# Attention's kv products in two blocks, its loads on one queue, the expert choice per batch, and token numbers from two engines

## The chip, the cores and the metric

The kernel runs on one core of a Trainium2 chip. The metric is the device time of one execution in microseconds (us); of several runs the median counts. Each compute engine (PE is TensorE, DVE is VectorE, ACT is ScalarE, POOL is GpSimd) and SP (SyncE) runs its own instruction stream in order; streams meet at semaphores. SP, ACT and POOL each have a DMA queue.

## The reference

The work has three parts: linear attention with a norm over each head, a mixture of experts in which every token takes its best expert, and a second one in which experts have a capacity and tokens are assigned by descending logit.

```python
# q, k, v: (8 batches, 8 heads, 576 rows, 64), float32
kv = np.einsum('bhsd,bhse->bhde', k, v)
out = np.einsum('bhsd,bhde->bhse', q, kv)
rms = np.sqrt(np.mean(out * out, axis=-1, keepdims=True) + 1e-06)
x = out / rms * g_norm                       # then (4608 tokens, 512)

# first mixture, 8 experts, 512 -> 1024 -> 512
logits = x @ w_gate
e_idx = np.argmax(logits, axis=1)
gate_w = softmax(logits)[np.arange(N), e_idx]
eom = 1.0 / (1.0 + np.exp(-(x @ w_output_gate)))
out[mask] = gate_w * eom[e] * (np.maximum(x[mask] @ w1[e], 0) @ w2[e])
# second mixture: the same shapes, at most N // 8 tokens an expert,
# tokens assigned greedily over all (token, expert) logits in descending order
```

## The kernel before

**Attention.** The rows of a batch lie on 96 partitions, six rows each (`CT = 6`). PE walks `STEPS_A = 56` steps; with `B = 8` batches, batch b's work begins in step 6b. In a step (lines 658 to 714) PE does in this order: a group of eight products k by v, 1/6 of the batch's kv (L670, profile name kv_ps, 16 matmul records, as each float32 product is two); in one step of six the gates of kv (L682, kt_ps, waits for ACT's kvT); the turning of a row tile of q, 7 steps behind (L692, qt_ps); the product of q with kv, 8 steps behind (L704, o_ps); in one step of six the turning of kv (L713, kt_ps, waits for ACT's copies of kv, L1001). So kv of batch b is made in steps 6b to 6b+5, its turning comes in step 6b+6, and its products with q in steps 6b+8 to 6b+13. In the text below, "step c of a batch" counts its products with q.

ACT per step: the copy of the turned q (L1007), the regrouping of the next q (L1015, named q), and, behind DVE's scaling of the product (xrow, L1207), the squares (L1027) and the copy of the raw logits (L1031). DVE: the scaling, the sums of squares (L1186), and once a batch the inverse root (L1225 to 1229), the scaled logits (lraw, L1240) and their sum (lgs, L1244). POOL then scales xrow in two runs of three instructions (L586) and stores each half to x_rows (L592). DVE's L1207 waits in steps 0 and 3 of a batch until the store of the same half two batches before has landed (L1206).

**Loads.** k and v of a batch come in halves of four heads, 576 KB each, into two buffers each; q comes in halves into three. SP issues the k halves and one q half (lines 470 to 475), waiting for the kv products that free the buffer; ACT issues the v halves and the other q half (L972 to 990), the first seven before its other work and the rest inside its steps. All go through `load_heads` (L459). Behind the last of them SP issues the first expert's weights (L493). ACT splits these weights after attention (`first_high`, L965).

**Routing.** After the last batch DVE takes, over all 48 row tiles (`G1`) at once, the largest logit (L1251), the shifted logits for ACT's exponentials (L1253), the one-hot choice with ties to the lower expert (L1255 to 1259), a running count (L1262), the gate factor (L1269 to 1274), and each token's slot in a list sorted by expert (L1279 to 1292). Then, in three equal thirds of 16 row tiles, it makes a one-hot of the slot's tile (oha1, L1296), two products of it with the two digits of the token number (ra1, L1299; 64 times the one plus the other), and a one-hot of the place within the tile (ohb and ohx, L1305 to 1308). PE multiplies these (L727), and DVE joins the digits to the token numbers tok_i and the mask cap_v (L1322 to 1326) and releases `s_route`. On it wait POOL's gathers of x (L604), SP, and PE's first mixture. Both mixtures follow; the change leaves them alone.

## Time and profile before

| what | us |
|---|---|
| median of 3 runs | 1430.93 |
| the runs | 1423.6 to 1432.06 |
| the profiled execution | 1435.5 |
| its span | 1433.8 |
| PE busy in the span | 1264.1 (88%) |
| DVE busy | 975.6 (68%) |
| ACT busy | 443.4 (31%) |
| POOL busy | 384.1 (27%) |

The span runs from the first to the last instruction of the one profiled execution; 1.7 us of that execution lie around it. All rows below come from it, with times counted from the span's start. A share of busy time is an average over attention, routing and two mixtures, which have different limits, so the rows below are taken from the first 230 us, where the change is.

### The profile page before, as it was taken

How to read it: one execution, taken by the hardware profiler on the slowest of the kernel's cores; microseconds unless marked ns; L12 is line 12 of the kernel's file. 1: busy time of each engine (PE TensorE's matmuls, PEld its weight loads, DVE VectorE, ACT ScalarE, POOL GpSimd, SP SyncE). 2: the span in 40 equal slices, each digit the busy share in tenths (PEclk: the TensorE clock that was granted, in tenths of full speed). 3: DMA queues.
4: the chain of work that ended last, by engine and by line, in shares of the span. 5: the costliest groups of instructions: out<-in, count | busy, mean ns of one | idle time of the engine just before them, and what ended most of it. 6: DMA issues, size and time to landing. Idle time of an engine off the chain costs nothing.

```text
span 1433.8 us, 21814 instructions
## 1 busy us (share of the span) xinstructions
PE 1264.1 (88%) x7584; PEld 1013.6 (71%) x7584; DVE 975.6 (68%) x2318; ACT 443.4 (31%) x801; POOL 384.1 (27%) x323
## 2 busy tenths in 40 slices
PE   5987925999799999999999317999999999999996
PEld 4876814788688888888888215677777777777884
DVE  1464696476576777777668787788888788886621
ACT  1665641222222222222222021232333333233421
POOL 2233442955460725436000001020211111111110
PEclk7899866999999999999999657999999999999998
DMA  9999224698331432433110031313232332314100
GB/s 212 229 284 306 83 71 162 230 341 294 95 124 49 151 110 90 154 88 127 45 38 23 15 117 34 125 56 129 75 125 90 108 102 84 133 59 145 47 30 19
DMA packets 71014, 172.07 MB, mean 120 GB/s; under 512 B 11752, under 2 KB 30264, under 8 KB 70272
## 3 DMA queue, kind: packets, MB, share of 16 engines
q1 hardware_dynamic: 37104, 94.45, 20.6%
q10 hardware_dynamic: 21696, 36.35, 9.1%
q0 software_dynamic: 12112, 39.87, 8.7%
q8 instruction: 68, 1.11, 0.3%
q14 instruction: 34, 0.28, 0.1%
HBM read 129.42 MB, written 41.23 MB: 119 GB/s over the span
## 4 chain that ended last, share of the span: by engine, by line
PE 70%; DVE 8%; DMA 8%; POOL 7%; issue 5%; ACT 1%; SPq 0%; POOLq 0%; ACTq 0%; DVEq 0%
PE bank L742 52%; PE bank L814 4%; PE bank L760 4%; DMA v_sb<-in_v 3%; POOL w_lo L578 3%; PE bank L870 2%; POOL xrow L586 2%; DMA xst<-x_rows,tok_i 2%; PE bank L807 2%; PE o_ps L704 1%; POOL w_hi L576 1%; DMA w_sb<-in_moe_w 1%; DMA x_rows<-xrow 1%; POOL xst L604 1%; PE bank L797 1%
## 5 line engine op out<-in xcount | busy, mean ns | idle before, releaser
L1386 DVE SCALAR_TENSOR_TENSOR bank<-bank,factor,wg2b 128x512 f32<-128x512 f32 x336 | 254.6, 758 | 10.4
L1352 DVE TENSOR_TENSOR hT_lo<-bank,hT_hi 128x512 fp32r<-128x512 f32 x150 | 96.5, 684 | 169.9 <-ACT hT_hi L1092 154.5
L1049 ACT ACTIVATE h<-bank 128x512 f32<-128x512 f32 x166 | 99.1, 598 | 320.3 <-PE bank L742 305.5
L742 PE MATMUL bank<-w_hi,xT_hi 128*128 (+1 forms) x600 | 175.7, 415 | 10.2 <-POOL w_lo L578 7.3
L742 PE MATMUL bank<-w_lo,xT_hi 128*128 (+1 forms) x600 | 174.3, 406 | 0.0
L633 POOL DMA_INDIRECT xg<-y_rows,gat_i x40 | 39.5, 987 | 495.4 <-DVE sca_i L1509 382.2
L742 PE MATMUL bank<-w_hi,xT_lo 128*128 (+1 forms) x600 | 168.1, 401 | 0.0
L742 PE MATMUL bank<-w_hi,hT_hi 128*128 (+1 forms) x600 | 160.9, 409 | 5.2 <-DVE score L1389 3.3
L742 PE MATMUL bank<-w_lo,hT_hi 128*128 (+1 forms) x600 | 158.2, 400 | 0.0
L742 PE MATMUL bank<-w_hi,hT_lo 128*128 (+1 forms) x600 | 155.7, 398 | 0.0
L578 POOL TENSOR_TENSOR w_lo<-w_sb,w_hi 128x1024 fp32r<-128x1024 f32 x56 | 134.2, 2396 | 4.5
L742 PEld LDWEIGHTS bank<-w_hi,xT_lo 128*128 128x128 f32 x600 | 113.4, 191 | 27.0
L742 PEld LDWEIGHTS bank<-w_lo,xT_hi 128*128 128x128 f32 x600 | 112.5, 191 | 26.6
L742 PEld LDWEIGHTS bank<-w_hi,hT_lo 128*128 128x128 f32 x600 | 111.7, 188 | 26.7
L742 PEld LDWEIGHTS bank<-w_hi,xT_hi 128*128 128x128 f32 x600 | 107.6, 192 | 31.3 <-issue 11.4
L742 PEld LDWEIGHTS bank<-w_lo,hT_hi 128*128 128x128 f32 x600 | 111.1, 189 | 25.5
L742 PEld LDWEIGHTS bank<-w_hi,hT_hi 128*128 128x128 f32 x600 | 109.3, 192 | 27.4 <-issue 6.7
L576 POOL CAST w_hi<-w_sb 128x1024 fp32r<-128x1024 f32 x56 | 58.2, 1040 | 182.6 <-DMA w_sb<-in_moe_w 182.6
L1056 ACT ACTIVATE y<-bank,factor 128x512 f32<-128x512 f32 x43 | 29.6, 687 | 216.5 <-PE bank L742 191.7
L814 PEld LDWEIGHTS bank<-ident,h 128*128 128x128 f32 x664 | 86.4, 190 | 7.6 <-ACT h L1049 0.4
L1092 ACT ACTIVATE hT_hi<-bank 128x512 fp32r<-128x512 f32 x150 | 81.5, 597 | 25.5 <-PE bank L814 16.0
L640 POOL DMA_INDIRECT out<-y,sca_i x40 | 39.8, 995 | 180.8 <-ACT y L1080 118.9
(257 smaller groups left out, 1809.3 us busy)
## 6 DMA issues: line engine op xcount, KB each, us to landing
w_sb<-in_moe_w SPq DMA_DIRECT2D x112, 512.0 KB, 7.6
y_rows<-y ACTq DMA_DIRECT2D x43, 256.0 KB
x_sorted<-xst SPq DMA_DIRECT2D x41, 260.0 KB
xg<-x_sorted ACTq DMA_DIRECT2D x41, 260.0 KB
k_sb<-in_k SPq DMA_DIRECT2D x16, 576.0 KB, 12.6
v_sb<-in_v ACTq DMA_DIRECT2D x16, 576.0 KB, 14.1
x_rows<-xrow POOLq DMA_DIRECT2D x16, 576.0 KB, 5.4
w_sb<-in_moe_w SPq DMA_DIRECT2D x4, 2048.0 KB, 14.4
```

What stands on the lines that cost most here:

```text
L576: pool.tensor_copy(w_hi[:, 1 - e % 2, cols(i)], w_sb[:, e % 2, cols(i)]).then_inc(s_phi, 1)
L578: pool.tensor_tensor(w_lo[:, e % 2, cols(i)], w_sb[:, e % 2, cols(i)], w_hi[:, 1 - e % 2, cols(i)].bitcast(F32), ALU.subtract).then_inc(s_ ...
L633: pool.indirect_dma_start(out=xgs[w % 2][0:rows, 0:DM], out_offset=None, in_=y_rows[:, :], in_offset=bass.IndirectOffsetOnAxis(ap=gat_i[0: ...
L640: pool.indirect_dma_start(out=out[:, :], out_offset=bass.IndirectOffsetOnAxis(ap=sca_i[0:rows, w:w + 1], axis=0), in_=ys[w % 2][0:rows, :] ...
L742: mm = pe.matmul(ps, a[:, i % chunks, :], b[:, i % chunks, cols], start=(i == 0), stop=(i == 3 * chunks - 1))
L760: mm = pe.matmul(ps[0:rows, :], act[:, c, 0:rows], w[rows < P][:, c, cols], start=(i == 0), stop=(i == 2 * chunks - 1))
L814: mm = pe.transpose(th_ps[half][:, i * P:(i + 1) * P], h[:, half * 4 + i:F:FC], ident[:, :])
L1049: act.activation(h[:, half * HALF:(half + 1) * HALF], h_ps[half][:, :], ACT.Copy if short else ACT.Relu).then_inc(s_h, 1)
L1056: act.activation(ys[t % 2][:, :], y1_ps[t % 2][:, :], ACT.Copy, scale=factor[:, t:t + 1]).then_inc(s_y, 1)
L1092: act.activation(hT_hi[:, half * 4:(half + 1) * 4, :].rearrange("p a b -> p (a b)"), th_ps[half][:, :], ACT.Copy).then_inc(s_hT, 1)
L1352: dve.tensor_tensor(hT_lo[:, half * 4:(half + 1) * 4, :].rearrange("p a b -> p (a b)"), th_ps[half][:, :], hT_hi[:, half * 4:(half + 1) * ...
L1386: ch.link(dve.scalar_tensor_tensor(out=prod_ps[:, :], in0=y1_ps[t % 2][:, :], scalar=factor[:, t:t + 1], in1=wg2b[:, e, :], op0=ALU.mult, ...
```

## The change

Four things change. (1) SP issues all loads of q, k and v in the order k, v, k, v, q, with q of a batch in one transfer of 1152 KB; ACT issues none. (2) After batch 0, the kv of batch b is made in two blocks of three groups, in steps 1 and 3 of the products of batch b - 1. (3) The largest logit, the shifted logits and the one-hot choice are made per batch in DVE's steps 4 and 5 behind its logits, on 6 row tiles at a time; the exponentials still run once, after the last batch. (4) Token numbers are split as (row of the partition, middle of the batch and step): one factor is a number per partition (row1), so ACT makes its product with a scaled copy, and DVE makes the other; the parts have 20, 16 and 12 row tiles; `s_route` is released behind tok_i, ahead of the mask.

```diff
+        MIDDLE = S * B // 2 - PT * CT // 2
...
-        payload1 = sb("payload1", [PT, G1, 2], F16)
+        payload1 = sb("payload1", [PT, G1], F16)
+        row1 = sb("row1", [PT, 1])
...
+        ROUTED = [slice(0, 20), slice(20, 36), slice(36, G1)]
+        N_CONST = 10
...
+        KV_BESIDE = ((), (0, 1, 2), (), (3, 4, 5), (), ())
+
+        def kv_steps(s):
+
+            if s < LAG_T:
+                return [(0, s)]
+            e, c = at_step(s, LAG_O)
+            return [(e + 1, i) for i in KV_BESIDE[c]] if e is not None and e + 1 < B else []
...
                     wait_pos(sp, s_kv, (b - 2) * 2 + n + 1)
-                    load_heads(sp, k, k_sb[b % 2], b, n, s_kvl[b % 2][n])
+                    for src, dst in ((k, k_sb), (v, v_sb)):
+                        sp.dma_start(dst[b % 2][:, n * half:(n + 1) * half, :],
+                                     src[b, n * half:(n + 1) * half].rearrange("h (p c) d -> p h (c d)", c=CT)
+                                     ).then_inc(s_kvl[b % 2][n], 16)
                 wait_pos(sp, s_q2, (b - 2) * CT)
-                load_heads(sp, q, q_sb[b % 3], b, 0, s_ql[b % 3])
+                sp.dma_start(q_sb[b % 3][:, :, :], q[b].rearrange("h (p c) d -> p h (c d)", c=CT)).then_inc(s_ql[b % 3], 16)
...
-                if b < B:
+                for b, i in kv_steps(s):
                     if i % 3 == 0:
                         pe.wait_ge(s_kvl[b % 2][i // 3], (b // 2 + 1) * 32)
...
-            for b in range(2):
-                for n in range(2):
-                    load_v(b, n)
-                load_q(b)
-            load_q(2)
             for s in range(STEPS_A + 1):
-                b, i = divmod(s, CT)
-                if i % 3 == 0 and 0 <= b - (i == 0) < B - 2:
-                    load_v(b + 2 - (i == 0), 1 - i // 3)
-                if i == 0 and 3 <= b + 1 < B:
-                    load_q(b + 1)
...
+            for n, gs in enumerate(ROUTED):
+                act.wait_ge(s_oha, n + 1)
+                act.activation(ra1[:, gs, :, 1], oha1[:, gs, :], ACT.Copy, scale=row1[:, 0:1]).then_inc(s_rar, 1)
             act.wait_ge(s_wgt, 1)
...
-            for s in range(STEPS_A + 4):
+            for s in range(STEPS_A + 6):
...
+                if e is not None and c >= 4:
+                    of = slice(e * CT, (e + 1) * CT)
+                    lg, mxb, part = lgs[:, of, 0:E], mx[:, of].unsqueeze(2).to_broadcast([PT, CT, E]), oh[:, of, :]
+                    if c == 4:
+                        dve.wait_ge(s_lgs, e + 1)
+                        link(dve.tensor_reduce(mx[:, of], lg, AX, ALU.max))
+                        ch.inc(dve.tensor_tensor(part, lg, mxb, ALU.is_equal))
+                        dve.tensor_tensor(sh[:, of, :], lg, mxb, ALU.subtract).then_inc(s_sh, 1)
+                        ch.wait()
+                        link(dve.tensor_tensor(part, part, rank8[0:PT, :].unsqueeze(1).to_broadcast([PT, CT, E]), ALU.mult))
+                    if c == 5:
+                        dve.wait_ge(s_sh, e + 1)
+                        link(dve.tensor_reduce(mx[:, of], part, AX, ALU.max))
+                        ch.inc(dve.tensor_tensor(onehot[:, :, of].rearrange("p e g -> p g e"), part, mxb, ALU.is_equal))
+                        link(dve.tensor_tensor(part, part, mxb, ALU.is_equal))
...
+                dve.wait_ge(s_oha, ROUTED.index(gs) + 1)
                 ch.wait()
...
+                dve.tensor_tensor(ra1[:, gs, :, 0], oha1[:, gs, :],
+                                  payload1[:, gs].unsqueeze(2).to_broadcast([PT, n_all, T1]), ALU.mult).then_inc(s_ohb, 1)
```

On PE, at the start of attention, before (kv_ps is the kv products, qt_ps the turned q, o_ps the product of q with kv, kt_ps the turned kv and its gates):

```order
0 L656 UNCONDITIONAL_BRANCH
1 L670 MATMUL kv_ps<-v_sb,k_sb 64x64 x56
2 L713 MATMUL kt_ps<-ident,kvgb 128x128 x4
3 L670 MATMUL kv_ps<-v_sb,k_sb 64x64 x8
4 L682 MATMUL kt_ps<-gate_bd,kvT 128x32 x4
5 L692 MATMUL qt_ps<-ident,q 128x96 x4
6 L670 MATMUL kv_ps<-v_sb,k_sb 64x64 x8
7 L692 MATMUL qt_ps<-ident,q 128x96 x4
8 L704 MATMUL o_ps<-kvgb,qT 96x160 x4
9 L670 MATMUL kv_ps<-v_sb,k_sb 64x64 x8
10 L692 MATMUL qt_ps<-ident,q 128x96 x4
```

And the same place now:

```order
1 L682 MATMUL kv_ps<-v_sb,k_sb 64x64 x48
2 L725 MATMUL kt_ps<-ident,kvgb 128x128 x4
3 L694 MATMUL kt_ps<-gate_bd,kvT 128x32 x4
4 L704 MATMUL qt_ps<-ident,q 128x96 x8
5 L716 MATMUL o_ps<-kvgb,qT 96x160 x4
6 L682 MATMUL kv_ps<-v_sb,k_sb 64x64 x24
7 L704 MATMUL qt_ps<-ident,q 128x96 x4
8 L716 MATMUL o_ps<-kvgb,qT 96x160 x4
9 L704 MATMUL qt_ps<-ident,q 128x96 x4
10 L716 MATMUL o_ps<-kvgb,qT 96x160 x4
11 L682 MATMUL kv_ps<-v_sb,k_sb 64x64 x24
```

The first kv group of batch 1 stood ahead of the turning of batch 0's kv; now the first product with q comes ahead of any kv of batch 1, and its groups stand in blocks of 24 products.

On DVE, behind the last logits, before (mx is the largest logit, sh the shifted ones, oh the one-hot in the making):

```order
184 L1244 TENSOR_REDUCE lgs<-lraw 96x96
185 L1251 TENSOR_REDUCE mx<-lgs 96x48
186 L1253 TENSOR_TENSOR sh<-lgs,mx 96x384
187 L1255 TENSOR_TENSOR oh<-lgs,mx 96x384
188 L1256 TENSOR_TENSOR oh<-oh,rank 96x384
189 L1257 TENSOR_REDUCE mx<-oh 96x48
190 L1258 TENSOR_TENSOR oh<-oh,mx 96x384
191 L1259 COPY onehot<-oh 96x384
192 L1262 SCALAR_TENSOR_TENSOR inc<-segment,onehot 96x384
```

And now:

```order
231 L1239 TENSOR_REDUCE lgs<-lraw 96x96
232 L1247 TENSOR_REDUCE mx<-lgs 96x6
233 L1248 TENSOR_TENSOR oh<-lgs,mx 96x48
234 L1249 TENSOR_TENSOR sh<-lgs,mx 96x48
235 L1251 TENSOR_TENSOR oh<-oh,rank 96x48
236 L1254 TENSOR_REDUCE mx<-oh 96x6
237 L1255 TENSOR_TENSOR onehot<-oh,mx 96x6x8
238 L1256 TENSOR_TENSOR oh<-oh,mx 96x48
239 L1259 SCALAR_TENSOR_TENSOR inc<-segment,onehot 96x384
```

Seven operations remain between the last logits and the running count, each on an eighth of the elements; the other seven batches' share lies in the steps of attention.

## Rows read from the trace of the kernel before

**Rows 1.** Stretches: PE, PEld, DVE, ACT, POOL busy us, granted clock, DMA share, GB/s.

```profile
20.00:40.00 20.00, 14.18 (x121) 12.78 (x122) 1.83 (x4) 7.06 (x14) 0.00 (x0) 0.66 1.10 229
76.00:78.00 2.00, 2.00 (x23) 1.73 (x22) 0.00 (x0) 0.00 (x0) 0.00 (x0) 1.00 1.03 406
160.00:180.00 20.00, 16.89 (x145) 14.94 (x144) 14.32 (x26) 13.47 (x34) 8.23 (x8) 0.91 0.21 61
```

**Rows 2.** Waits of 0 to 240 us: total us, times, longest.

```profile
DVE xrow L1207 <- DMA x_rows<-xrow: 12.7, 2, 8.8
...
ACT L1001 <- issue: 20.9, 1, 20.9
PE kv_ps L670 <- DMA v_sb<-in_v: 20.5, 4, 8.7
```

**Rows 3.** PE in order of time: start, us, instructions, in brackets its wait.

```profile
15.26 3.94 PE L670 MATMUL kv_ps<-v_sb,k_sb 96*64 96x64 f32 x48 [2.56 <-DMA v_sb<-in_v]
25.82 1.57 PE L670 MATMUL kv_ps<-v_sb,k_sb 96*64 96x64 f32 x16 [6.62 <-DMA v_sb<-in_v]
27.32 1.12 PE L713 MATMUL kt_ps<-ident,kvgb 128*128 128x128 f32 x4
...
36.58 0.97 PE L670 MATMUL kv_ps<-v_sb,k_sb 96*64 96x64 f32 x16
...
93.89 0.93 PE L670 MATMUL kv_ps<-v_sb,k_sb 96*64 96x64 f32 x16
...
96.31 0.97 PE L670 MATMUL kv_ps<-v_sb,k_sb 96*64 96x64 f32 x16
...
106.84 0.66 PE L713 MATMUL kt_ps<-ident,kvgb 128*128 128x128 f32 x4 [0.64 <-ACT kvgb L1001]
...
108.35 1.08 PE L682 MATMUL kt_ps<-gate_bd,kvT 128*128 128x32 f32 x8
...
110.81 0.93 PE L670 MATMUL kv_ps<-v_sb,k_sb 96*64 96x64 f32 x16
```

**Rows 4.** Batch 7's steps, which have no kv beside them, in order of time.

```profile
175.37 1.63 PE L704 MATMUL o_ps<-kvgb,qT 128*96 128x160 f32 x8
...
179.08 0.69 DVE L1207 TENSOR_TENSOR xrow<-o_ps,g_sb 96x512 f32<-96x512 f32 x1 [0.55 <-PE o_ps L704]
...
181.51 0.55 PE L692 MATMUL qt_ps<-ident,q 96*128 96x96 f32 x4
...
186.43 1.33 PE L704 MATMUL o_ps<-kvgb,qT 128*96 128x160 f32 x8 [0.59 <-ACT qT L1007]
```

**Rows 5.** DMA: packets at 24 to 34 us; q1 (SP's) at 105 to 107; a store at 124.

```profile
DMA packets 1540, 2.30 MB, mean 230 GB/s; under 512 B 54, under 2 KB 1539, under 8 KB 1539
...
q1 hardware_dynamic: 321, 0.47, 101.9%
...
x_rows<-xrow POOLq DMA_DIRECT2D x1, 576.0 KB, 15.6
```

**Rows 6.** Behind attention, in order of time.

```profile
193.29 1.46 DVE L1244 TENSOR_REDUCE lgs<-lraw 96x96 f32<-96x768 f32 x1
...
197.08 3.57 DVE L1256 TENSOR_TENSOR oh<-oh,rank 96x384 f32<-96x384 f32 x1
197.17 3.05 POOL L586 TENSOR_TENSOR xrow<-xrow,rin 96x512 f32<-96x512 f32 x3
...
199.73 0.52 ACT L1039 ACTIVATE ex<-sh 96x384 f32<-96x384 f32 x1
...
202.38 0.95 DVE L1262 TENSOR_TENSOR_SCAN inc<-segment,onehot 96x384 f32<-96x384 f32 x1
...
204.50 0.54 DVE L1269 TENSOR_REDUCE se<-ex 96x48 f32<-96x384 f32 x1
...
210.48 0.87 DVE L1296 TENSOR_TENSOR oha<-iota,slot 96x688 f16<-96x688 f32 x1
211.38 1.72 DVE L1299 TENSOR_TENSOR ra<-oha,payload 96x688 f16<-96x688 f16 x2
```

More of the change, by code:

```diff
@@ L468, in _ @@
         def _(sp):
+            half = H // 2
             for b in range(B):
@@ L566, in _ @@
                            allow_small_or_imprecise_dtypes=True))
-            made(pool.iota(ids_i[:, :], pattern=[[S, B], [1, CT]], base=1, channel_multiplier=CT))
+            made(pool.iota(ids_i[:, :], pattern=[[S, B], [1, CT]], base=-MIDDLE, channel_multiplier=0))
+            made(pool.iota(row1[:, :], pattern=[[0, 1]], base=1, channel_multiplier=1, allow_small_or_imprecise_dtypes=True))
             made(pool.iota(slots_i[:, :, 0:1], pattern=[[1, T1]], base=0, channel_multiplier=0))
@@ L724, in _ @@
             for g in range(G1):
-                if g % (G1 // 3) == 0:
-                    pe.wait_ge(s_ohb, g // (G1 // 3) + 1)
+                for n, gs in enumerate(ROUTED):
+                    if g == gs.start:
+                        pe.wait_ge(s_ohb, n + 1)
+                        pe.wait_ge(s_rar, n + 1)
                 mm = pe.matmul(bank[2][:, 0:2 * T1], ohb[0:PT, g, :] if g < T1 else ohx[:, g - T1, :],
@@ L1041, in _ @@
             act.activation(ez[:, :], zs[:, :], ACT.Exp, scale=-1.0).then_inc(s_ez, 1)
+            for n, gs in enumerate(ROUTED):
+                act.wait_ge(s_oha, n + 1)
+                act.activation(ra1[:, gs, :, 1], oha1[:, gs, :], ACT.Copy, scale=row1[:, 0:1]).then_inc(s_rar, 1)
             act.wait_ge(s_wgt, 1)
@@ new lines, in _ @@
+            for gs in ROUTED:
+                n_all = gs.stop - gs.start
+                n_main = min(gs.stop, T1) - gs.start
+                dve.tensor_tensor(oha1[:, gs, :], iota[0:PT, 0:T1].unsqueeze(1).to_broadcast([PT, n_all, T1]),
+                                  slot[:, 1, gs].unsqueeze(2).to_broadcast([PT, n_all, T1]), ALU.is_equal).then_inc(s_oha, 1)
+                iob = iota[0:PT, :].unsqueeze(1)
+                if n_main < n_all:
+                    ch.inc(dve.tensor_tensor(ohx[:, 0:n_all - n_main, :], iob.to_broadcast([PT, n_all - n_main, P]),
+                                             slot[:, 2, T1:gs.stop].unsqueeze(2).to_broadcast([PT, n_all - n_main, P]),
+                                             ALU.is_equal))
+                ch.inc(dve.tensor_tensor(ohb[0:PT, gs.start:gs.start + n_main, :], iob.to_broadcast([PT, n_main, P]),
+                                         slot[:, 2, gs.start:gs.start + n_main].unsqueeze(2).to_broadcast([PT, n_main, P]),
+                                         ALU.is_equal))
+                dve.wait_ge(s_oha, ROUTED.index(gs) + 1)
+                ch.wait()
+                dve.tensor_tensor(ra1[:, gs, :, 0], oha1[:, gs, :],
+                                  payload1[:, gs].unsqueeze(2).to_broadcast([PT, n_all, T1]), ALU.mult).then_inc(s_ohb, 1)
@@ L1322, in _ @@
             link(dve.tensor_copy(ids[:, :, :].rearrange("p a b -> p (a b)"), bank[2][:, 0:2 * T1]))
[L1323 to L1326 removed]
+            link(dve.scalar_tensor_tensor(out=idf[:, :], in0=ids[:, :, 1], scalar=float(CT), in1=ids[:, :, 0], op0=ALU.mult, op1=ALU.add))
+            dve.tensor_scalar(tok_i[:, :], idf[:, :], float(MIDDLE - CT), None, ALU.add).then_inc(s_route, 1)
+            link(dve.tensor_scalar(cap_v[:, :], ids[:, :, 1], 1.0, 0.5, ALU.min, ALU.subtract))
+            link(dve.tensor_scalar(cap_v[:, :], cap_v[:, :], 2 * MASKED, None, ALU.mult))
             dve.wait_ge(s_route, 1)
```

58 lines of the change are left out of this document (7 added, 51 removed).

## The prediction

> **What bounds the kernel now.** I read first the table of 20 us stretches, then the waits up to 240 us, then the instructions in order of time around each wait, and the DMA queues last, because a full DMA share alone does not say who waits. The stretches show two different early kernels. At 20 to 40 us the DMA share is 1.10 at 229 GB/s: the loads of q, k and v keep all DMA engines occupied. At 160 to 180 us the share is 0.21 and PE, DVE and ACT are all fairly busy: there it is the chain of attention itself that takes the time [rows 1]. The waits say what the full DMA costs: ACT cannot begin its work for 20.9 us, because it is issuing loads; PE waits 20.5 us in four pieces for v; DVE waits 12.7 us for stores of x_rows to free a buffer [rows 2].
>
> One undisturbed batch of six steps takes 110.81 - 93.89 = 16.92 us on PE, almost without gaps: per step one kv group of 16 matmuls (0.93 us), the turning of q and the product with kv, 2.42 together from one kv group's start to the next (93.89 to 96.31), so the turning of kv and its gates cost 16.9 - 6 x 2.42 = 2.4 us more once a batch [rows 3]. But from the kv group that starts at 36.58 (step 1 of batch 0) to the product at 175.37 (end of step 0 of batch 7, the same place but for one product) [rows 3, 4] are 138.8 us for seven batches, 19.8 each. Some 20 us are thus lost to waits and to the lower clock after them, before the last product starts at 186.43 [rows 4].
>
> Behind attention, DVE alone works on the routing; nothing large runs beside it, and everything of the first mixture waits for the token numbers at its end. So a microsecond taken off there should reach the end whole.
>
> **The loads on one queue.** After the change SP issues all 16 k, 16 v and 8 q transfers, ACT none. Would one queue be slower than two? At 24 to 34 us, with both queues full, 1540 packets move, 154 per us. At 105 to 107 us the SP queue is alone: 321 packets in 2 us, 160 per us, 234 GB/s [rows 5]. One queue with transfers waiting is as fast as two. I take 0 for the bandwidth; the bounds from these rows are plus and minus 4%, which is under 1 us at the start, where alone loads decide. ACT gets back its issue instructions and, above all, its start.
>
> **The start.** The kv of batch 0 is done at 15.26 + 3.94 = 19.2 us [rows 3]. Before, PE then stood at the first kv step of batch 1 until that batch's half landed (25.82), with the turning of kv, the gates and the first products queued behind it. Now that kv step is moved behind the first product of batch 0. From the turning of kv (27.32) to the kv group of step 9 (36.58) PE took 9.26 us, of which two kv groups at the low clock (1.57 each) are gone; 6.1 us remain [rows 3]. ACT, free now, copies kv at 19.3 and perhaps loads its table first, so the turning starts at 20.1 to 21.4 and step 9 at 26.2 to 27.5. The first half of batch 1 landed at 25.8 before, so it is just there. I take 27.5 instead of 36.58: 9 us earlier. Less of it would be left if the half came later; the bound is 5.
>
> **The batch with kv in two blocks.** Now step 1 and step 3 of a batch hold three kv groups each (3 x 0.93 = 2.8 us) and the other four none. PE's work is the same, 14.5 plus the turning, but the overlap changes. Without a kv group the chain decides: from DVE's scaling of a product (179.08) to the turning of the q that ACT made behind it (181.51) are 2.43 us, then a step's own 2.42 - 0.93 = 1.5, with handovers 1.6, so some 4.1 for two steps [rows 4]. I walk one batch from the start of the first block: step 1 is 2.8 + 1.6 = 4.4. Step 2 finds its q ready (ACT worked under the block): 1.6, at 6.0. Step 3 has the other block: 4.4, at 10.4. Step 4: 1.6, at 12.0. Its turning of kv waits for ACT's two copies of kv, which stand behind its work of step 3, and starts at 12.7; from there to the gates are 106.84 to 108.35 = 1.5 us [rows 3], so the gates start at 14.2 and, with 1.08 for them, step 5 ends at 16.8. Step 0 of the next batch: 1.6. The batch takes 18.4 us, 1.5 longer than the undisturbed 16.9 and 1.4 shorter than the 19.8 that it really took. I add 0.3 for handovers that the walk leaves out: 18.7. The bounds are 16.9 (all hidden) and 22 (both blocks 4.4, each of the four other steps held for a whole chain of 2.43, and 3.5 around the turning of kv).
>
> Do the loads keep up? A batch loads 3.54 MB, 15.1 us at 234 GB/s, and stores 1.18 MB; while stores run, 406 GB/s move (76 to 78 us) [rows 1], so a store adds little. A batch needs less than 17 us of DMA against 18.7 of walk, and its halves are needed two to three steps later than before. The waits for v go away and PE's chain becomes the bound.
>
> **The sum for attention.** First block at 27.5; first batch 18.7 + 3 for the low clock that rows of before show until 36 us: 49. Six more batches: 49 + 6 x 18.7 = 161. Batch 7 has no kv beside it; from its step 0 to its last product before were 186.43 - 175.37 = 11.1 us, of which 1.2 lie before my mark, the end of that step 0's product: 171. Stores: one issued at 124 us, beside the large weight pieces, took 15.6 us to land [rows 5]. The walk leaves some 8 us from the issue of a store to the step that needs its buffer; a wait there up to 1.9 us falls under the next kv block and is free, so I count only the one beside the weights, 2 us (0 to 8). The choice of the first expert for batch 6 adds seven short DVE operations to the last two steps, 1 us. So the last product starts at 174: 12 us earlier (5 to 20).
>
> **The choice per batch.** Before, from the end of the logits at 194.76 to the scan at 202.38 are 7.6 us on the critical chain, with 3.57 us for one product: GpSimd's three products run from 197.17 to 200.22, and DVE's ends 0.43 behind them [rows 6]. After it, seven operations on 96x48 remain behind the last logits, six handovers at about 0.2 us: 1.5. But then DVE meets GpSimd's second run with the scan or the last comparison instead; if that blocks it to the end of the run, the scan ends 1.9 us earlier and not 6. From the other side ScalarE limits: behind its splitting of the first weights, which stays where it is, come the table load and the exponentials, which end at 200.25; so DVE's sum of them, at 204.50 before, can't come more than 4.2 us earlier [rows 6]. I take 3.5 (1.8 to 4.2).
>
> The Trainium skill (SBUF — State Buffer, section "Who interferes with whom") says that a VectorE instruction with two inputs in SBUF contends with a GpSimd instruction that reads SBUF, and that the loser is blocked for that whole instruction. The trace agrees on who is blocked, but its 3.57 us spans the run of three GpSimd instructions, not one of about 1 us. By the rule taken for one instruction the saving would stand at its upper bound; by the row nearer to its lower one. Neither changes more than 1.2 us of the sum.
>
> **The token numbers.** Per third DVE did one comparison (0.87), two products (1.72) and a wide comparison [rows 6]. One of the two products goes to ScalarE, which is idle and has the whole wide comparison's time for it: 3 x 0.86 = 2.6 us less. The unequal parts (20, 16, 12) only change where it lies. The last part leaves PE 12 products behind DVE instead of 16, but DVE's small operations for the tile table hide both: 0. The token numbers no longer wait for the mask: 0.3. I take 2.9 (2.2 to 3.3). SP's store of the turned router comes later, behind ScalarE's third product, and still before the route: 0. The new iota of POOL and DVE's two operations less fall under the first load: 0.
>
> **Sum.** 12 + 3.5 + 2.9 = 18.4 off the profiled execution: 1435.5 - 18.4 = 1417.1. That execution was 4.6 above the median of the runs (1430.93), so the median becomes 1412.5; I say 1413. What a measurement of this kernel can tell from no change is about 1%, 14.3 us, so the line is at 1416.6.
>
> **Rivals.** *The blocks give the gain back.* If a batch takes 20.5 to 22 instead of 18.7, 6 x 1.8 to 6 x 3.3 = 11 to 20 us are lost: 1424 to 1433. For it: the chain of 2.43 us in the tail [rows 4], and DVE's extra work per batch in the steps where it already has the longest; against: ACT works under the block. Chance 0.17, nearly all within 1%.
> *The stores bind as before.* The waits for x_rows stay (12.7 us) or grow, since their deadline moves nearer: 8 us less gain, 1420. For it: 15.6 us beside the weights [rows 5], against: one queue less to share with. Chance 0.16; 0.06 faster, 0.10 the same.
> *The clock falls.* Slower. PE, gapless today in a batch, gets two gaps of about 1 us at the turning of kv. After the waits for v the granted clock was 0.66 over 20 to 40 us [rows 1], and a kv group took 1.57 us instead of 0.93 [rows 3]. If it stays at the lower level (1.2 GHz) throughout, the 16.3 us of work per batch become about 26, and the seven batches cost 7 x 7.6 = 53 more: 1466. From about a third of the stretch on it takes the whole gain (18.4 of 53), from two thirds on the kernel is slower by over 1%. Against: behind the wait of 0.64 us at 106.84 the same batch went on and ended in 16.9 us [rows 3]. Chance 0.06.
> *More than I count* (no store wait, a batch at 17.5): 1402. Chance 0.06.
> *The forecast*, 1405 to 1421: 0.55, of which 0.44 is faster by over 1%. Together: faster 0.56, same 0.37, slower 0.07. The range goes from 1402 to 1427.
>
> **What would show it.** In the changed profile: ACT's first copy at 19 to 21 us and the first product at about 26; PE's blocks of 48 in periods of 18 to 19 us; waits for v nearly gone while the rate of loads stays at 230; the last product at 170 to 178; between the last logits and the scan's end 2.5 us if GpSimd doesn't block and 6.7 if it does, instead of 8.6; 2.6 us less for the three parts. I am wrong if the blocks come in periods over 21 us, if PE waits for v again, or if the time gained before the route is lost behind it.

## The result, and the profile after

The changed kernel takes 1419.97 us, the median of its ten runs, beside 1428.18 us for the kernel before on the same chip (1423.55 to 1432.06). Nine of the ten lie at 1413.81 to 1422.12, one was disturbed (3983.54), and the ratio that follows leaves it out. The ratio is 0.9944, with a 95% interval of 0.9921 to 0.9968. That is 0.6% faster, within the 1% that the prediction called no change. Forecast were 1413 us and 1402 to 1427 for the range; the likeliest class, faster by over 1%, did not come.

The profiled execution of the changed kernel took 1422.12 us, its span 1420.4. That is 13.4 us less than the 1435.5 of the kernel before, while the medians differ by 8.2. The executions profiled stand at different places in their ranges: that of before is 7.3 us above its new median, that of after 2.2. Indeed that of before was slower than each of the ten runs of before beside it, and that of after was the slowest of its nine. Marks along the way show where the 13.4 us arose:

| mark, us from the span's start | before | after | gained so far |
|---|---|---|---|
| step 9's kv group / first block | 36.58 | 26.79 | 9.8 |
| last product starts | 186.43 | 176.79 | 9.6 |
| end of the logits | 194.75 | 187.14 | 7.6 |
| end of the scan | 203.33 | 193.80 | 9.5 |
| slots known, first comparison | 210.48 | 200.94 | 9.5 |
| end of the three parts | 225.28 | 212.96 | 12.3 |
| GpSimd's first gather | 229.42 | 216.80 | 12.6 |
| end of the span | 1433.8 | 1420.4 | 13.4 |

The busy shares hardly differ (PE 89%, DVE 69%, ACT 31%, POOL 27%). The stretches of the changed kernel answer to [rows 1], in the same columns.

```profile
20.00:40.00 20.00, 17.61 (x176) 15.56 (x173) 5.79 (x10) 9.90 (x24) 0.00 (x0) 0.83 1.10 235
140.00:160.00 20.00, 13.85 (x124) 13.01 (x123) 6.89 (x15) 5.53 (x14) 7.53 (x8) 0.66 0.53 199
160.00:180.00 20.00, 13.15 (x96) 10.77 (x94) 17.29 (x37) 13.07 (x33) 7.53 (x7) 1.00 0.15 47
```

PE works 3.4 us more at 20 to 40 us, since the first products come earlier, and the loads' rate on one queue is 235 GB/s, not less than 229. But at 140 to 160 us PE stands still for 6 of 20 us, and the granted clock is 0.66. The waits up to 240 us of the changed kernel, beside [rows 2]:

```profile
PEld qt_ps L704 <- ACT q L1010: 19.5, 23, 6.4
...
DVE xrow L1202 <- DMA x_rows<-xrow: 13.8, 4, 7.3
PE qt_ps L704 <- ACT q L1010: 13.1, 8, 6.2
...
PE kv_ps L682 <- DMA v_sb<-in_v: 10.2, 2, 8.3
```

The waits for v are halved: the two left are those for batch 0. The waits for the stores of x_rows have not gone: four instead of two, 13.8 us instead of 12.7. Where the longest is, PE's rows in order of time show (the first product; then from batch 6's gates to batch 7's last product):

```profile
24.52 2.34 PE L716 MATMUL o_ps<-kvgb,qT 128*96 128x160 f32 x8
...
134.81 1.08 PE L694 MATMUL kt_ps<-gate_bd,kvT 128*128 128x32 f32 x8 [0.86 <-ACT kvT L1016]
...
138.91 2.48 PE L682 MATMUL kv_ps<-v_sb,k_sb 96*64 96x64 f32 x48
...
149.10 0.90 PE L704 MATMUL qt_ps<-ident,q 96*128 96x96 f32 x4 [6.15 <-ACT q L1010]
149.80 2.34 PE L716 MATMUL o_ps<-kvgb,qT 128*96 128x160 f32 x8
152.07 4.28 PE L682 MATMUL kv_ps<-v_sb,k_sb 96*64 96x64 f32 x48
...
162.77 1.08 PE L694 MATMUL kt_ps<-gate_bd,kvT 128*128 128x32 f32 x8 [0.86 <-ACT kvT L1016]
...
176.79 1.33 PE L716 MATMUL o_ps<-kvgb,qT 128*96 128x160 f32 x8 [0.59 <-ACT qT L1002]
```

What to see here is a period, from one batch's gates to the next: 162.77 - 134.81 = 27.96 us, where the one before took 17.56 (117.25 to 134.81). PE waits 6.15 us for a q that ACT makes only behind DVE's scaling, which waits for a store. DVE's row and ACT's behind it:

```profile
146.38 0.69 DVE L1202 TENSOR_TENSOR xrow<-o_ps,g_sb 96x512 f32<-96x512 f32 x1 [7.27 <-DMA x_rows<-xrow]
...
147.10 0.59 ACT L1022 ACTIVATE sq<-o_ps 96x512 f32<-96x512 f32 x1 [7.36 <-DVE xrow L1202]
```

Behind the wait the block of 48 takes 4.28 us instead of 2.48 and a product 2.34 instead of 1.25: the granted clock is 0.50 at 146 to 154 us, the lower level, 1.2 GHz.

### The profile page after: what moved, and what is told of

Its sections match the earlier page's. It is cut to its first block, busy times and chain, and to the rows that moved or that the text cites. A ratio compares the mean times of both kernels' runs of the same rounds, so it can differ in the third digit from the quotient of the medians.

```text
span 1420.4 us, 21868 instructions
## 1 busy us (share of the span) xinstructions
PE 1258.0 (89%) x7584; PEld 1008.6 (71%) x7584; DVE 983.9 (69%) x2361; ACT 446.4 (31%) x804; POOL 386.0 (27%) x324
## 4 chain that ended last, share of the span: by engine, by line
PE 71%; DVE 8%; POOL 8%; DMA 7%; issue 5%; ACT 1%; SPq 0%; POOLq 0%; ACTq 0%; DVEq 0%
PE bank L756 53%; PE bank L828 4%; PE bank L774 4%; POOL w_lo L591 3%; POOL xrow L599 2%; DMA xst<-x_rows,tok_i 2%; PE bank L884 2%; PE bank L821 2%; DMA x_sorted<-xst 1%; PE kv_ps L682 1%; POOL w_hi L589 1%; PE o_ps L716 1%; DMA w_sb<-in_moe_w 1%; PE bank L811 1%; DMA x_rows<-xrow 1%
## 5 line engine op out<-in xcount | busy, mean ns | idle before, releaser
L1382 DVE SCALAR_TENSOR_TENSOR bank<-bank,factor,wg2b 128x512 f32<-128x512 f32 x336 | 254.7, 758 | 10.4
## 6 DMA issues: line engine op xcount, KB each, us to landing
v_sb<-in_v SPq DMA_DIRECT2D x16, 576.0 KB, 18.8
```

Source lines behind the costliest of these rows:

```text
L1382: ch.link(dve.scalar_tensor_tensor(out=prod_ps[:, :], in0=y1_ps[t % 2][:, :], scalar=factor[:, t:t + 1], in1=wg2b[:, e, :], op0=ALU.mult, ...
```

## The experiments

In each kernel the period is the time from one batch's gates (L682 before, L694 after) to the next batch's, seven of them; "store wait" is DVE's wait for x_rows. Ratios are to the kernel before, which was timed anew beside each of three groups of kernels; its medians there were 1426.06 us (first four kernels), 1426.76 (late_weights, before_late, four_pieces, pool_apart) and 1426.39 (the others). Each kernel has one profile, of one execution. Behind GpSimd's first gather, where no edit changes the work, these executions differ by up to 6.2 us (1198.2 to 1204.4 to the end of the span), so a difference between two spans says less than one between two marks.

**One part at a time.** Four kernels, each the kernel before with one part of the change.

one_queue, loads alone:

```
-                    load_heads(sp, k, k_sb[b % 2], b, n, s_kvl[b % 2][n])
+                    for src, dst in ((k, k_sb), (v, v_sb)):
+                        sp.dma_start(dst[b % 2][:, n * half:(n + 1) * half, :],
...
-                    load_v(b, n)
-                load_q(b)
```

> The kernel before, with only the loads moved: SP issues all of q, k and v, ScalarE none; kv stays one group a step. Theory (the gain of attention needs the loads and the blocks together: the kv step of batch 1 still stands ahead of the first product, so PE waits there for that half until 25.8 us as before): the kv group of step 9 starts at 34 to 37 us (36.58 before), the last product within 3 us of 186.43, the time within 3 us. Rival A (ScalarE's loads alone held the start): step 9 at 28 us, the last product at 177 to 179, the time 8 us less. Rival B (two queues load faster than one): the rate at 20 to 40 us under 220 GB/s, the last product later than 188.

Measured: 1423.12 us, ratio 0.9979 (0.9956 to 1.0003). The first gates came at 29.20 us (29.90 before) and step 9's kv group at 36.20: the start did not move, as the theory has it. The rate at 20 to 40 us was 236 GB/s, so rival B falls. But the last product started at 175.05, 11.4 us earlier than in before's profile, in spite of a store wait of 4.9 us; the theory had it within 3, and rival A only with an early start. What was wrong is what I compared with; numbers_alone shows it.

two_blocks, the order of kv alone:

```
-                b, i = divmod(s, CT)
...
-                if b < B:
+                for b, i in kv_steps(s):
```

> The kernel before, with only kv put in two blocks a batch (steps 1 and 3), the loads still on two queues. Theory (blocks are needed later than single groups, and the first product no longer stands behind batch 1's half, but ScalarE issues loads until its first copy): first block at 29 to 33 us, the blocks' period 17.5 to 19 us, the last product at 179 to 183, the time 4 to 7 us less. Rival A (the blocks by themselves bring nothing, the free ScalarE does): the last product within 2 us of 186.43. Rival B (the blocks alone bring it all): the last product at 176 to 178, the time 8 to 10 us less.

Measured: 1427.68 us, ratio 1.0005 (0.9971 to 1.0039). The first block came at 32.05 us and the last product at 182.83, in the theory's ranges. But the periods were 17.5 to 23.1 us, 20.5 in the mean, not 17.5 to 19, though the execution had only one store wait, of 2.5 us. Its granted clock was 0.83 at 60 to 100 us and 0.91 at 100 to 140. The time misses the 4 to 7 us: blocks alone save nothing by the runs.

choice_alone, the choice per batch alone:

```
-            link(dve.tensor_reduce(mx[:, :], lg, AX, ALU.max))
...
+                if e is not None and c >= 4:
+                    of = slice(e * CT, (e + 1) * CT)
...
+                        link(dve.tensor_reduce(mx[:, of], lg, AX, ALU.max))
```

> The kernel before, with only the first expert chosen per batch inside attention. Theory (a comparison held through GpSimd's run of three products takes most of the gain, and batch 6's choice delays the last steps): from the end of the last logits to the end of the scan 6.7 us instead of 8.58, from the last product to the end of the logits 1 to 2 us more than 8.3; the time within 1.5 us of before. Rival (what was forecast: 3.5 us on the choice and 1 us lost): the time 2.5 us less.

Measured: 1428.33 us, ratio 1.0004 (0.9971 to 1.0038). From the end of the logits (194.96) to the end of the scan (201.59) are 6.63 us instead of 8.58, and from the last product (184.61) to the end of the logits 10.35 instead of 8.32. The one takes 2.0 us off and the other puts 2.0 on: as the theory said, nothing is left.

numbers_alone, the token numbers alone:

```
-                for w in range(2):
-                    ch.inc(dve.tensor_tensor(ra1[:, gs, :, w], oha1[:, gs, :],
...
+                dve.tensor_tensor(ra1[:, gs, :, 0], oha1[:, gs, :],
...
+                act.activation(ra1[:, gs, :, 1], oha1[:, gs, :], ACT.Copy, scale=row1[:, 0:1])
```

> The kernel before, with only the token numbers' change (one of two products on ScalarE, parts of 20, 16 and 12, the route released before the mask). Theory: from the first comparison for the tile numbers to the end of the last part 12.1 us instead of 14.9, to GpSimd's first gather 3.0 to 3.2 us less than 18.94, and all of it reaches the end: the time 3 us less (1425 beside 1428). Rival (the time saved ahead of the first gather is lost behind it, since weights and stores set what follows): 0 to 1 us less.

Measured: 1422.81 us, ratio 0.9987 (0.9958 to 1.0016). These are its DVE's and POOL's rows behind the route's slots, beside [rows 6]:

```profile
201.04 1.05 DVE L1303 TENSOR_TENSOR oha<-iota,slot 96x860 f16<-96x860 f32 x1
...
213.07 0.15 DVE L1318 TENSOR_SCALAR ends_i<-cnt 1x8 int32<-1x8 f32 x1
```

```profile
216.90 1.54 POOL L609 DMA_INDIRECT xg<-x_rows,tok_i  x1 [25.10 <-DVE tok_i L1330]
```

The parts take 12.03 us instead of 14.80, and the gather comes 15.86 us behind the first comparison instead of 18.94: 3.1 us, as expected. The runs' 0.13% has an interval too wide to tell 3 us from 0. (The four ratios together make 0.25% less, the whole change 0.56%; with intervals of about 0.3% either way on each that is no contradiction, and no proof that the parts add up.) The surprise lies elsewhere. This kernel's attention is that of the kernel before, instruction for instruction, and yet its last product started at 176.95 us, 9.5 earlier than 186.43. In its execution DVE's wait for the store that was issued near the weights was this:

```profile
142.62 0.69 DVE L1214 TENSOR_TENSOR xrow<-o_ps,g_sb 96x512 f32<-96x512 f32 x1 [1.18 <-DMA x_rows<-xrow]
```

In before's it was 8.8 us [rows 2], in choice_alone's 7.96. So an unchanged attention takes 177 or 186 us, by the execution. (The profile of numbers_alone, 1419.06 us, is the fastest of its kernel's ten runs, and that of before, 1435.5, lies among the slowest of its own, so the 9.5 us are near the extremes.) In before and choice_alone the first store of batch 4 was issued at 124 and 123 us, behind the weights (123.6 and 121.5), and took 15.6 and 14.9 us to land; in numbers_alone it was issued at 122, ahead of the weights (123.75), and took 7.3. The order of issue is not the whole of it: with one queue the weights are issued well ahead of that store in each profile (at 114 to 120 us, the store at 132 to 140), and it took 8.4 us in four_pieces, 11.1 in one_queue, 11.8 in pool_apart and 14.1 in the changed kernel.

**The store beside the weights.** late_weights is the changed kernel with this:

```
             for n in range(2):
+                sp.wait_ge(s_xst[n], 16 * (B - 2))
+            for n in range(2):
                 load_half(0, n, s_wl)
```

> The changed kernel; SP issues the two loads of the first weights only when the stores of x_rows of batches 0 to 5 have landed. Theory (a store beside the 16 KB packets of the weights takes 14 to 17 us instead of 8 to 9, DVE waits 7.3 us for it in batch 7, and the half clock behind that adds some 3): the stores of batch 5 land in 7 to 10 us, the last period between gates is 17.5 to 19 us instead of 27.96, the last product starts at 166 to 169 instead of 176.79, the time is 8 to 10 us less than the changed kernel's (1410). Rival A (the wait only moves: slots come free no earlier, loads of batch 7 hold PE): the last product within 2 us of 176.79. Rival B (the weights come too late and hold ScalarE's split of them behind the last logits): the last product early, but the scan's end no earlier than 193.8.

(The stores in question are those of batch 4, which batch 6's scaling waits for; the added wait asks for those of batch 5 too, so it comes later than needed.) Measured: 1412.29 us in four runs, ratio 0.9899 (0.9852 to 0.9947). PE's rows in order of time show its last gates, and the DMA view at 133 to 134 us the store that took 14.1 us in the changed kernel (under it the time to landing, above it what the loads' queue still moves):

```profile
118.56 1.08 PE L696 MATMUL kt_ps<-gate_bd,kvT 128*128 128x32 f32 x8 [0.86 <-ACT kvT L1018]
...
136.09 1.08 PE L696 MATMUL kt_ps<-gate_bd,kvT 128*128 128x32 f32 x8 [0.86 <-ACT kvT L1018]
...
153.61 1.08 PE L696 MATMUL kt_ps<-gate_bd,kvT 128*128 128x32 f32 x8 [0.86 <-ACT kvT L1018]
...
167.63 1.33 PE L718 MATMUL o_ps<-kvgb,qT 128*96 128x160 f32 x8 [0.59 <-ACT qT L1004]
```

```profile
q1 hardware_dynamic: 69, 0.09, 30.6%
...
x_rows<-xrow POOLq DMA_DIRECT2D x1, 576.0 KB, 4.2
```

The last period is 17.52 us instead of 27.96 and the last product starts at 167.63, 9.2 us earlier; the span is 1406.8, 13.6 less than in the changed kernel's profile (the fastest of four runs beside the slowest of nine). Rivals A and B fall: nothing else took the wait's place, and the scan ended at 184.66. Of the profile's gain the medians, each set against the kernel before beside it, show 0.45%, 6.4 us, and the two intervals overlap a little. For the changed kernel the DMA view of the stretch in which the store was to land (136 to 146 us) has these lines:

```profile
DMA packets 433, 4.18 MB, mean 418 GB/s; under 512 B 36, under 2 KB 36, under 8 KB 225
...
q1 hardware_dynamic: 227, 3.39, 79.5%
q0 software_dynamic: 205, 0.77, 19.2%
```

The weights' queue holds 79.5% of the engines' time in fewer than half the packets (3.39 MB in 227), the store's queue 19.2% in 205. The Trainium skill (DMA: Bandwidth & Descriptors, section "Queues, rings and completion order") says that a DMA engine takes turns between queues packet by packet. The trace agrees: packets are shared almost evenly, 205 to 227, and bytes are not.

before_late is the same wait in the kernel before.

> The kernel before with the same wait ahead of the first weights. Theory (in the kernel before the long store wait comes or not by chance: 8.8 us in one execution, 1.2 in the one of numbers_alone, by whether batch 5's first store is issued before the weights' packets flow): the last product at 174 to 178, the time 3 to 6 us under before's median, and the spread of its runs narrower than before's 15 us. Rival (the spread of before has another source): median within 1.5 us, spread as before.

Measured: 1424.82 us, ratio 0.9995 (0.9969 to 1.0021); its runs went from 1416.78 to 1431.08, those of before from 1420.04 to 1436.12. In the trace the long wait is gone as expected (three of 2.8 to 3.2 us earlier in attention stay; last period 16.6). The last product starts at 169.60, earlier than the 174 to 178 expected, but this profile is the fastest of its ten runs (span 1415.0). But the median moved by 1.9 us only, within the interval, and the spread stayed: the rival. The chance wait is real in single executions, but it is not what spreads the runs of the kernel before.

before_late and late_weights also show the change without the store wait on either side. The last product starts at 169.60 and 167.63, 2.0 us apart; the logits end at the same time (177.93 and 178.00); the scan ends 1.9 us earlier and the first gather comes 4.9 us earlier (212.59 and 207.65). So in this pair attention brings next to nothing, and the token numbers and the choice bring what there is up to the gather. The medians differ by more, 12.5 us; what makes up the rest no mark in the first 230 us shows (behind the gather the two profiles differ by 3.3 us).

**Blocks against single groups.** four_pieces is the changed kernel with smaller pieces:

```
-        KV_BESIDE = ((), (0, 1, 2), (), (3, 4, 5), (), ())
+        KV_BESIDE = ((0,), (1, 2), (3,), (4, 5), (), ())
```

> The changed kernel with kv in pieces of 1, 2, 1 and 2 groups at steps 0, 1, 2 and 3 instead of two blocks of 3 at 1 and 3. Theory (the early start comes from kv of batch 1 standing behind the first product, not from the blocks; the blocks cost 0.6 to 1 us a batch, 17.5 against 16.6 to 16.9 undisturbed): the first gates at 21 us as in the changed kernel, undisturbed periods of 16.7 to 17.2, the last product 2 to 5 us earlier than 176.79. Rival (blocks let ScalarE and DVE work ahead, single groups don't): periods of 18 or more, the last product later than 177.

Measured: 1418.59 us, ratio 0.9935 (0.9904 to 0.9966). Undisturbed periods were 17.65, not 16.7 to 17.2; the last product started at 175.15. The piece size does nothing; theory and rival both miss. What costs the 0.6 to 0.9 us is then not the block. My reading is this: with single groups the next batch's kv stood between the turning of kv and the gates and covered the wait for ACT's copy (no bracket at 108.35 in [rows 3]); in both new orders nothing stands there, and PE waits 0.86 us. That is argued from the rows: no run moved it alone.

singles_late is late_weights with kv in single groups as in the kernel before (the other three parts of the change kept):

> The changed kernel with the late weights, but kv one group a step as in the kernel before. Theory (the early start of the blocks, 8 us, is given back over seven batches, since a batch with blocks takes 17.5 us undisturbed and one with single groups 16.6 to 17.1): the first gates at 29 us instead of 21.67, all seven periods 17.0 to 18.5, the last product at 166 to 171 beside 167.63 of late_weights, the time within 3 us of it. Rival (the blocks' early start reaches the end): the last product at 174 to 176, the time 7 us more than late_weights.

Measured: 1414.28 us, ratio 0.9910 (0.9879 to 0.9940), beside 0.9899 of late_weights. Its last rows of the same kind:

```profile
134.40 1.08 PE L688 MATMUL kt_ps<-gate_bd,kvT 128*128 128x32 f32 x8
...
151.00 1.23 PE L688 MATMUL kt_ps<-gate_bd,kvT 128*128 128x32 f32 x8 [0.86 <-ACT kvT L1010]
...
166.55 1.33 PE L710 MATMUL o_ps<-kvgb,qT 128*96 128x160 f32 x8 [0.59 <-ACT qT L996]
```

It starts 7.4 us later (gates at 29.03 against 21.67) and ends attention 1.1 us earlier (166.55 against 167.63): its seven periods take 122.0 us, those of late_weights 131.9. The early start of the blocks is given back whole, at 1.4 us a batch. That is more than the 0.6 to 0.9 us between undisturbed batches of either kind; the rest goes with stretches at the lower clock (in three of the seven periods of late_weights a product behind the gates takes over 2 us) and store waits of 2.4 and 2.8 us in two more. The runs can't tell the two kernels apart. The theory holds, though two of the periods (16.6 and 16.8) lie under its 17.0.

**GpSimd and the choice.** pool_apart is the changed kernel with a wait of GpSimd for its own last product:

```
                                        ALU.mult).then_inc(s_xn, 1)
+                    pool.wait_ge(s_xn, b * CT + c + 1)
```

> The changed kernel; GpSimd waits for each of its products before it starts the next, so they don't stand back to back. Theory (DVE's instruction with two inputs is held until a run of GpSimd's products ends, because they follow each other without a gap): the comparison that took 3.73 us (L1255) takes at most 1.3, no instruction of DVE behind the last logits takes over 1.5, from the logits' end to the scan's end 4 to 5 us instead of 6.66. Rival A (DVE is held as long as GpSimd works, gap or not): 3.7 to 4.5 us for one instruction again. Rival B (held once by each product): several instructions of 1 us each, and the scan's end no earlier than 6 us behind the logits. The time 0 to 2 us less.

Measured: 1417.24 us, ratio 0.9935 (0.9913 to 0.9957). First DVE behind the last logits in the changed kernel, with GpSimd's run, then DVE in pool_apart:

```profile
187.54 1.07 DVE L1249 TENSOR_TENSOR sh<-lgs,mx 96x48 f32<-96x48 f32 x1
...
189.00 3.73 DVE L1255 TENSOR_TENSOR onehot<-oh,mx 96x48 f32<-96x48 f32 x1
...
192.85 0.95 DVE L1259 TENSOR_TENSOR_SCAN inc<-segment,onehot 96x384 f32<-96x384 f32 x1
```

```profile
189.58 3.05 POOL L599 TENSOR_TENSOR xrow<-xrow,rin 96x512 f32<-96x512 f32 x3
```

```profile
184.50 1.07 DVE L1252 TENSOR_TENSOR oh<-oh,rank 96x48 f32<-96x48 f32 x1
...
185.84 0.24 DVE L1256 TENSOR_TENSOR onehot<-oh,mx 96x48 f32<-96x48 f32 x1
...
186.20 2.48 DVE L1260 TENSOR_TENSOR_SCAN inc<-segment,onehot 96x384 f32<-96x384 f32 x1
188.71 0.83 DVE L1262 COPY tot<-inc 96x8 f32<-96x8 f32 x1
```

The comparison (L1255, here L1256) takes 0.24 us instead of 3.73, and the scan ends 4.8 us behind the logits instead of 6.66: with gaps in GpSimd's run the long hold is gone. But the scan is held instead (2.48 for 0.95), though less; why the gaps did not free it stays open. From the logits' end to the slots are 12.60 us instead of 13.80, and from the scaling of the last product but one to the logits' end 9.94 instead of 9.70: 1.0 us in all. The theory's bound of 1.5 us for one instruction is broken by the scan, and the 1.0 us can't be told from 0 in the runs.

**More room for the stores, and a shorter tail.** five_halves is late_weights with five half buffers for x_rows instead of two whole ones:

```
-            xrow = [sbe(f"xrow{i}", [PT, CT, DM]) for i in range(2)]
+            xhalf = [sbe(f"xrow{i}", [PT, CT // 2, DM]) for i in range(4)]
...
+            xhalf.append(sbe("xrow4", [PT, CT // 2, DM]))
...
-                        wait_pos(dve, s_xst[c // 3], (e - 1) * 16)
+                        dve.wait_ge(s_xst[(m - 5) % 2], ((m - 5) // 2 + 1) * 16)
```

> late_weights with x_rows staged in five half buffers instead of two whole ones, so that a store has half a batch more to land. Theory (the periods of 19 instead of 17.5 come from DVE's waits of 1.1 to 2.8 us for stores, which take 9 us beside the loads): no wait of DVE for x_rows, all periods from the second 17.5 to 17.9, the last product at 159 to 163 instead of 167.63, the time 5 to 8 us under late_weights (1405). Rival (the loads then bind: 3.54 MB a batch at 234 GB/s and the stores beside them): PE waits for v or ScalarE for q instead, periods 18.5 to 19, the time within 2 us of late_weights.

(ScalarE's split of the first weights also waits for a store of batch 6 here, a wait that late_weights has not.) Measured: 1409.92 us, ratio 0.9881 (0.9850 to 0.9912). There is no store wait left, and four periods in a row are 17.5. But the first two are 21.2 and 19.0, and the last is 19.0, though PE waits for no store there: the gates' gaps of 0.59 and 0.86 us are followed by products of 2.21 and 1.70 us, the granted clock is 0.64 at 134 to 138 us. So a part of what I had put down to stores is the lower clock. The last product starts at 165.03, 2.6 us earlier and not 4.6 to 8.6, and the two medians can't be told apart: the theory's mechanism holds, its size was half wrong.

five_pieces is five_halves with the smaller pieces of four_pieces:

> five_halves with kv in pieces of 1, 2, 1 and 2 groups at steps 0 to 3 instead of two blocks. Theory (in four_pieces undisturbed periods were 17.65, no shorter than with blocks, 17.5): the last product within 1.5 us of that of five_halves, the time within 2 us. Rival (smaller pieces leave fewer gaps): periods of 16.9, the time 3 us less.

Measured: 1408.91 us, ratio 0.9885 (0.9855 to 0.9915), the last product at 166.83, undisturbed periods 17.65. No difference that a run can tell; the last product misses the 1.5 us by 0.3.

five_last_two is five_halves with the choice of batches 6 and 7 made in one pass behind the last logits:

```
-                if e is not None and c >= 4:
-                    of = slice(e * CT, (e + 1) * CT)
+                if e is not None and c >= 4 and e != B - 2:
+                    n = 2 if e == B - 1 else 1
+                    of = slice((e + 1 - n) * CT, (e + 1) * CT)
```

> five_halves with the choice of batch 6 left to that of batch 7 (one pass over both behind the last logits). Theory (seven operations of batch 6 and a hold by GpSimd's products stand between the last two products' scaling, and cost 2.0 us of the tail): from the last product to the logits' end 8.4 to 8.9 us instead of 10.35, the choice 0.3 to 0.6 longer, the time 1 to 2 us under five_halves. Rival (the steps' end is set by the squares and ScalarE, not by DVE's order): no change in the tail.

Measured: 1403.81 us, ratio 0.9851 (0.9820 to 0.9883), the best of all kernels: 1.5% under the kernel before.

```profile
162.66 1.33 PE L719 MATMUL o_ps<-kvgb,qT 128*96 128x160 f32 x8 [0.60 <-ACT qT L1007]
```

```profile
169.54 1.46 DVE L1245 TENSOR_REDUCE lgs<-lraw 96x96 f32<-96x768 f32 x1
...
173.08 3.67 DVE L1262 TENSOR_TENSOR onehot<-oh,mx 96x96 f32<-96x96 f32 x1
...
176.89 0.95 DVE L1266 TENSOR_TENSOR_SCAN inc<-segment,onehot 96x384 f32<-96x384 f32 x1
```

From the last product to the logits' end are 8.34 us instead of 10.36, and from there to the scan's end 6.84 instead of 6.66: 1.8 us gained, as expected. The medians differ by 6 us from five_halves, more than the edit explains by the trace, with intervals that overlap; that this is the best kernel is thus clear against the kernel before, not against five_halves.

## Why the prediction was right and where it was wrong

The median, 1420.0, lies in the range and in the forecast's own band (1405 to 1421), at its upper end, and not in the class forecast as likeliest. That it lies inside that band is partly luck: the kernel before came out 2.7 us faster than in its three earlier runs, and at their median of 1430.93 the measured ratio would have given 1423. The working was right in fewer places than the number makes it look.

*Loads on one queue, cost 0.* Right: 235 GB/s with one queue, 236 in one_queue, 229 with two (222 in two_blocks).

*The start.* The first block came at 26.79 us, forecast 27.5. The step that failed is the one behind it, that the 9 us reach the last product. singles_late starts 7.4 us later than late_weights and ends attention 1.1 us earlier. The rival "the blocks give the gain back" had the right mechanism and a chance of 0.17; it needed no batch of 20.5 us for it, only single groups that run faster than the 19.8 us I took them for (16.6 to 18.4 us a batch in singles_late; with two queues, in before_late, 16.6 to 18.6 behind a first of 19.7).

*The batch, 18.7 us.* From the first gates to the seventh, 21.02 to 134.81, are 19.0 us a batch: near, but for other reasons. Undisturbed the batch takes 17.5, not 18.7: the walk took a block as 3 x 0.93 = 2.8 us, and from its start to the next instruction are 2.40 (121.36 to 123.76), 0.8 less a batch. The rest is store waits and stretches at the lower clock. I had called a wait up to 1.9 us free under a kv block, and the one of 1.2 us was (its period is 17.56); those of 2.4 and 3.0 us lie in periods of 18.8 and 19.4, and the sum had no such wait outside the weights.

*The store beside the weights, 2 us (0 to 8).* The worst-sized term in this profile. Its period is 10.4 us longer than the undisturbed one, outside the bounds, and late_weights, which takes it away, has 17.52. In pool_apart and four_pieces the same wait is 5.4 and 1.5 us, so its size varies with the execution or with the small edits there. I had the 15.6 us of the store in [rows 5] before me, and bounded the wait only by the walk's slack; the half clock behind a wait of that size, 1.8 us on one block alone, had no place in the sum.

*The baseline of attention.* The 19.8 us a batch of the kernel before came from one execution with an 8.8 us store wait. numbers_alone runs the same attention and starts the last product at 176.95 (169.60 in before_late, whose weights come late). So 12 us were counted against a starting point that other executions beat by 9 and more. That the profiled execution was 4.6 us above the median was taken off at the end, but no term was made smaller for it: the 18.4 us were carried over whole. In the profile pair the term looks good, 9.6 us for 12. Of the 18.4 us forecast the pair shows 13.4 and the medians 8.2: 5.0 are missing in the terms of the pair (attention 2.4, the tail behind the last product 2.0, the choice 1.6, less 1.0 gained in the token numbers and behind the gather), and 5.2 are the places of the two profiled executions in their ranges (7.3 and 2.2 us above the medians). That the kernel before now has a median of 1428.2 and not 1430.9 gave 2.7 of them back, and 7.5 us are left between 1412.5 and 1420.0. How much of the 5.2 is the long store wait is not shown: before_late takes it away and the median moves by 1.9.

*The tail, 1 us for batch 6's choice.* 2.0 us (10.35 against 8.32 in choice_alone, 8.34 when it is taken out again in five_last_two).

*The choice, 3.5 us (1.8 to 4.2).* 1.9 us: 6.66 against 8.58. The text named this case, 6.7 if GpSimd blocks, and took a value in the middle. The comparison was held 3.73 us beside GpSimd's run. The Trainium skill (SBUF — State Buffer, section "Who interferes with whom") calls the shared port pair an exclusive lock and says, of VectorE's two-port modes, that the engine that comes second is blocked for the other's whole instruction; one instruction of about 1 us does not cover 3.73, the run of three (3.05 us, until 192.63) does, and pool_apart, where only the gaps in the run differ, brings it to 0.24. Choice and tail together are nothing, and the runs of choice_alone say the same.

*The token numbers, 2.9 us.* Right: 2.8 for the parts, 3.1 to the first gather, and in the profile pair no part of it is lost behind (12.6 us at the gather, 13.4 at the end).

*Clock.* No fall throughout, but local falls in some batches behind the gates, where the new order has its two gaps, some 1.4 us each (periods of 18.96 beside 17.5); this rival was put as all or nothing. That the gaps bring the falls is not shown, since most batches have the same gaps and no fall.

*Open.* What spreads the runs of one kernel over 5 to 16 us is not found: the chance wait is not it, by before_late. The slower runs have the lower mean granted clock (0.929 to 0.938 for the slowest three of the 25 runs of before beside late_weights, 0.944 to 0.946 for the fastest three), which may be cause or effect. Whether it differs between kernels, and so what a profile's 1 or 2 us are worth in a median, stays open as well.

## What to carry to other kernels

A stage's length read from one profiled execution is one draw: before a gain is counted against it, look whether it holds a wait whose length changes from execution to execution, and put the sum against a stage without it. A large load with long packets that starts while a buffer's store is still needed is a case of its own: hold it back until the store has landed, if nothing needs it early (here 9 us in the profiles and 6 in the medians of the changed kernel, with intervals that overlap; in the kernel before nothing that the runs could tell). And a head start in a pipelined loop is worth only what the period leaves of it; compare the periods first.

## What the runs showed of the hardware that was not expected

- A store of 576 KB from GpSimd's queue lands in 4.1 to 4.2 us where little else is under way (the last eight stores in before), in 6.3 to 10.7 beside the loads of q, k and v, and in 14.1 to 17.0 for the two stores behind the issue of the weights in before, choice_alone (14.9 and 15.5) and the changed kernel (14.1 and 14.5), whose loads move about 15 KB a packet (3.39 MB in 227). In other executions stores that met the weights took 5.1 to 11.8.
- The hold of a two-input instruction of VectorE by GpSimd lasted as long as GpSimd's products followed each other without a gap: 3.73 us beside three. With a wait between them none was over 1.1 on an operation of 96x48, but a scan of 0.95 took 2.48.
- Gaps of only 0.59 and 0.86 us on PE are followed in some batches, and not in others, by products at half clock (2.21 us instead of 1.25).
